# RWKV attention, soft MoE and FFN in one kernel: the low weights to GpSimd, the opening of the FFN in another order

## The chip, the cores and the metric

The kernel runs on one core of a Trainium2 chip. The metric is device microseconds of one launch; the median of three runs of the kernel before is 386.32 us (386.26 to 386.83).

## What is computed

Three layers follow each other. The first is a linear attention with a decaying state (4 batches, 8 heads, 768 tokens, head size 48), the second a soft mixture of 8 experts with 4 slots each, the third a feed-forward layer:

```python
y[t]   = r[t] @ (state + (u * k[t]) outer v[t]);  state = w * state + k[t] outer v[t]
logits = x @ phi;  d = softmax over tokens;  c = softmax over slots
slot_out[e] = relu((d.T @ x)[e] @ w1[e]) @ w2[e]
x2     = c @ slot_out                      # 3072 tokens x 384
h      = x2 @ w_in;  g = h * sigmoid(1.702 * h);  out = g @ w_out    # 384 -> 2048 -> 384
```

## The kernel before, in words

Each engine has its own instruction list, written out by hand; they meet only through semaphores, each of which counts up. An instruction that waits holds everything behind it on its engine. The first 120 us are the attention, in 6 chunks of 128 tokens by 4 batches; the experts follow until about 154 us; the rest is the FFN, which is what the change touches.

The FFN is not computed as `(c @ slot_out) @ w_in`. The 32 slot rows are first multiplied with `w_in`, which gives a matrix M of 2048 columns (spread over 128 rows as `mst`), and then `hidden(i, f)` (L569) is one 128x512 matmul of `mst`'s block f (128 of the 2048 hidden columns, 16 blocks) with the weights `ct` of token tile i (512 tokens, 6 tiles). The operands of the FFN's matmuls have the type fp32r; each is split into a high part (a copy in that type) and a low part (the difference to the fp32 value), and the products are summed. For each block f of each tile i:

- TensorE: `hidden(i, f)` writes bank f % 4.
- ScalarE: `sigmoid(i, f)` (L1046) writes `sg`.
- VectorE: `product(i, f)` (L850) multiplies bank and `sg` to `gf` (two buffers).
- ScalarE: `high(i, f)` (L1052) copies `gf` to `ghi`. VectorE: `low(i, f)` (L857) subtracts to `glo` (four buffers each).
- TensorE: `product(i, f)` (L576) adds nine matmuls to three output banks: `whi` x `glo`, `whi` x `ghi`, `wlo` x `ghi` for each of three column blocks m.

TensorE runs `LEAD` = 3 hidden blocks ahead of the product. ScalarE's list runs `sigmoid(f)` ahead of `high(f - 1)`, VectorE's `product(f)` ahead of `low(f - 1)`.

The output weight is split in the same way while tile 0 runs, in nine parts (`PARTS`, L36: blocks 0, 1, then pairs 2-3, 4-5 ... 14-15): `high_wout(part)` (L1034) on ScalarE writes `whi`, `low_wout(part)` (L872) on VectorE writes `wlo` from the loaded weight and `whi`. TensorE waits for `wlo_ok` ahead of the product of every even block of tile 0 (L649).

The opening of tile 0 is written out by hand (L604 to L644 on TensorE, L882 to L907 on VectorE, L1071 to L1095 on ScalarE). M of the first 256 columns is made first (L608) with its own high and low part (L1073, L885, `mf_ok`), so that `hidden(0, 0)` and `hidden(0, 1)` can go before the whole of M is there; then M of all columns (L613: three k, each of four column tiles; `m_ps` at the end), then a few warm-up matmuls (`keep_warm`, L331) and `opening()`, the product of block 0 with its `wlo` part last (L591). Four pairs of matmuls (L630, L631) spread M over the batches' rows; four copies turn them into `mst` in SBUF, quarters 0 and 2 on ScalarE (L1063, `mst_even`), quarters 1 and 3 on VectorE (L877, `mst_odd`). `hidden(0, 2)` follows, then `product(0, 1)` with `hidden(0, 3)` let in ahead of its last column block by the argument `within`, then `tile(0)` (L646) from f = 2: `hidden(0, f + 3)`, then `product(0, f)`.

GpSimd's last work before the change is `spr` (L1180), at 135.8 us.

Of the kernel before, what the change touches and what calls it, by code (L numbers as in the profile page):

```python
# [8 lines left out]
ALU = mybir.AluOpType  # L9
# [10 lines left out]
KD = DM // P  # L20
# [4 lines left out]
KF = FF // P  # L25
# [10 lines left out]
PARTS = ((0, 1), (1, 2)) + tuple((k, k + 2) for k in range(2, KF, 2))  # L36
# [5 lines left out]
LEAD = 3  # L42
# [3 lines left out]
def wait(eng, sem, value):  # L46

    if not isinstance(value, int) or value > 0:
        eng.wait_ge(sem, value)


def rwkv_soft_moe_ffn(nc, rk, kr, v, wcol, u, phi, w1, w2, win, wout, ident, strict, match, jsel, sel, parts, out):
    with ExitStack() as ctx:
        place = {"at": (nc.sbuf_base + 31) // 32 * 32}

        def sb(name, shape, dt=F32):
            size = 4
            for n in shape[1:]:
                size *= n
            t = nc.alloc_sbuf_tensor_at(name, shape, dt, offset=place["at"])  # L60
            place["at"] += (size + 31) // 32 * 32
            return t

        def sem(name):
            return ctx.enter_context(nc.semaphore(name))
# [91 lines left out]
        whi = sb("whi", [P, KF, DM], F32R)  # L157
        assert place["at"] == ring_at + 4 * SLOT_W * WLO_AT
        wlo = sb("wlo", [P, KF, DM], F32R)

        bank = [ctx.enter_context(nc.psum_tensor(f"bank{i}", [P, 512], F32)) for i in range(3)]
# [38 lines left out]
        own_ok, te_ps, spr_made, cturn_ps, chi_ok, clo_ok, mst_ps, mst_even, mst_odd = (  # L200
            sem(n) for n in ("own_ok", "te_ps", "spr_made", "cturn_ps", "chi_ok", "clo_ok", "mst_ps", "mst_even", "mst_odd"))
        rmax_ok, csub_ok, cexp_ok, rsum_ok, c_ok, ct_ps, ct_ok, whi_ok, wlo_ok = (
            sem(n) for n in ("rmax_ok", "csub_ok", "cexp_ok", "rsum_ok", "c_ok", "ct_ps", "ct_ok",
                             "whi_ok", "wlo_ok"))
# [12 lines left out]
        wraw = ring[:, WOUT_AT:WOUT_AT + 2, :].rearrange("p a n -> p (a n)").rearrange("p (k n) -> p k n", k=KF)  # L217
# [110 lines left out]
        def _(pe):  # L328
            pe.wait_ge(s_ident, 16)

            def keep_warm(to, count):  # L331

                for _ in range(count):
                    pe.matmul(to[:, 0:P], idt[:, :], idt[:, :], start=True, stop=True)  # L334
# [234 lines left out]
            def hidden(i, f):  # L569
                q = KF * i + f  # L570
                wait(pe, gf_ok, q - 3)
                pe.matmul(HB[f % 4][:, :], mst[:, f * P:(f + 1) * P],  # L572
                          ct_flat[:, bass.ds(i * TT, TT)],
                          start=True, stop=True).then_inc(hh_ps, 1)

            def product(i, f, within=None):  # L576
                q = KF * i + f
                pe.wait_ge(glo_ok, q + 1)
                hi, lo = ghi[:, f % 4, :], glo[:, f % 4, :]
                for m in range(KD):  # L580
                    if within and m == KD - 1:
                        within()
                    if f == 0:
                        wait(pe, o_ok, KD * (i - 1) + m + 1)
                    o = bank[4 + m][:, :]
                    w_hi, w_lo = whi[:, f, m * P:(m + 1) * P], wlo[:, f, m * P:(m + 1) * P]
                    pe.matmul(o, w_hi, lo, start=(f == 0), stop=False)  # L587
                    pe.matmul(o, w_hi, hi, start=False, stop=False)  # L588
                    pe.matmul(o, w_lo, hi, start=False, stop=(f == KF - 1)).then_inc(prod_ps, 1)  # L589
# [21 lines left out]
            for k in range(KD):  # L611
                for q in range(4):
                    last = pe.matmul(LG[32 * q:32 * q + 32, :], sot[:, k, :],  # L613
                                     win_sb[:, k, 512 * q:512 * q + 512], start=(k == 0), stop=(k == KD - 1))
                if k == 0:
                    pe.wait_ge(mf_ok, 1)
                    hidden(0, 0)
                    hidden(0, 1)
# [1 line left out]

            pe.wait_ge(ct_ok, B + 2)
            pe.wait_ge(spr_made, B)
            keep_warm(bank[2], 3)
            opening()
            pe.wait_ge(mhi_ok, 1)
            pe.wait_ge(mlo_ok, 1)
# [6 lines left out]
            pe.wait_ge(mst_odd, 1)  # L633
            hidden(0, 2)
            pe.wait_ge(wlo_ok, 2)

            def third():
                pe.wait_ge(mst_odd, 2)
                hidden(0, 3)

            product(0, 1, third)
            pe.wait_ge(mst_even, 2)
            for f in range(4, 2 + LEAD):
                hidden(0, f)  # L644

            def tile(i, more):  # L646
# [17 lines left out]
        def _(dve):  # L664
# [185 lines left out]
            def product(i, f):  # L850
                q = KF * i + f
                dve.wait_ge(sg_ok, q + 1)
                wait(dve, ghi_ok, q - 1)
                wait(dve, glo_ok, q - 1)
                dve.tensor_tensor(gf[:, f % 2, :], bank[f % 4][:, :], sg[:, f % 2, :], ALU.mult).then_inc(gf_ok, 1)  # L855

            def low(i, f):  # L857
                q = KF * i + f
                dve.wait_ge(ghi_ok, q + 1)
                wait(dve, prod_ps, KD * (q - 3))  # L860
                dve.tensor_tensor(glo[:, f % 4, :], gf[:, f % 2, :], ghi[:, f % 4, :], ALU.subtract)\  # L861
                   .then_inc(glo_ok, 1)
# [6 lines left out]
                    else:  # L869
                        low(i - 1, KF - 1)  # L870

            def low_wout(part):  # L872
                dve.wait_ge(whi_ok, part + 1)
                k = slice(*PARTS[part])
                dve.tensor_tensor(wlo[:, k, :], wraw[:, k, :], whi[:, k, :], ALU.subtract).then_inc(wlo_ok, 1)

            def copied(q):  # L877
                dve.wait_ge(mst_ps, q + 1)
                dve.tensor_copy(mst[:, 512 * q:512 * q + 512].rearrange("p (g k c) -> p g k c", g=2, k=2),
                                bank[MB[q]][:, :].rearrange("p (g c k) -> p g k c", g=2, k=2)).then_inc(mst_odd, 1)  # L880
# [3 lines left out]
            low_rows = mst[64:P, 0:FIRST].rearrange("p (k c) -> p k c", k=2)  # L884
            dve.scalar_tensor_tensor(low_rows, bank[5][64:P, 0:FIRST].rearrange("p (c k) -> p k c", k=2), rden[64:P, :],  # L885
                                     low_rows, ALU.mult, ALU.subtract).then_inc(mf_ok, 1)
            low_wout(0)
            low_wout(1)
            product(0, 0)
            product(0, 1)  # L890
            low(0, 0)
# [1 line left out]
            dve.scalar_tensor_tensor(mhl[:, 1, :], LG[:, :], rden, mhl[:, 0, :], ALU.mult, ALU.subtract)\  # L893
               .then_inc(mlo_ok, 1)
            low(0, 1)
            low_wout(2)
            copied(1)
            copied(3)
            product(0, 2)
            low(0, 2)  # L900
            low_wout(3)
            product(0, 3)
            for f in range(4, KF):
                product(0, f)
                low(0, f - 1)
                if f % 2 and f // 2 + 2 < len(PARTS):
                    low_wout(f // 2 + 2)  # L907
            with dve.Fori(1, C) as i:
                tile(i)
            low(C - 1, KF - 1)  # L910
# [3 lines left out]
        def _(act):  # L914
# [119 lines left out]
            def high_wout(part):  # L1034
                act.wait_ge(wout_in[PARTS[part][0] // QK], 16)
                k = slice(*PARTS[part])
                act.activation(whi[:, k, :], wraw[:, k, :], ACT.Copy).then_inc(whi_ok, 1)
# [8 lines left out]
            def sigmoid(i, f):  # L1046
                q = KF * i + f
                act.wait_ge(hh_ps, q + 1)
                wait(act, gf_ok, q - 1)
                act.activation(sg[:, f % 2, :], bank[f % 4][:, :], ACT.Sigmoid, scale=1.702).then_inc(sg_ok, 1)  # L1050

            def high(i, f):  # L1052
                q = KF * i + f
                act.wait_ge(gf_ok, q + 1)
                wait(act, prod_ps, KD * (q - 3))
                act.activation(ghi[:, f % 4, :], gf[:, f % 2, :], ACT.Copy).then_inc(ghi_ok, 1)  # L1056
# [6 lines left out]
            def copied(q):  # L1063

                g = slice(1 if q == 0 else 0, 2)
                act.wait_ge(mst_ps, q + 1)
                act.activation(mst[:, 512 * q:512 * q + 512].rearrange("p (g k c) -> p g k c", g=2, k=2)[:, g, :, :],
                               bank[MB[q]][:, :].rearrange("p (g c k) -> p g k c", g=2, k=2)[:, g, :, :], ACT.Copy)\
                   .then_inc(mst_even, 1)
# [11 lines left out]
            act.wait_ge(m_ps, 1)  # L1081
            act.activation(mhl[:, 0, :], LG[:, :], ACT.Copy, scale=rden).then_inc(mhi_ok, 1)
            high(0, 1)
            high_wout(2)
            copied(0)
            copied(2)
            sigmoid(0, 2)
            high(0, 2)
            high_wout(3)
            sigmoid(0, 3)  # L1090
            for f in range(4, KF):
                sigmoid(0, f)
                high(0, f - 1)
                if f % 2 == 0 and f // 2 + 2 < len(PARTS):
                    high_wout(f // 2 + 2)  # L1095
            with act.Fori(1, C) as i:
                for f in range(KF):
                    sigmoid(i, f)
# [83 lines left out]
                    .then_inc(spr_made, 1)  # L1182


# [57 lines left out]
```

## Time and profile before

| what | value |
|---|---|
| median of 3 runs | 386.32 us |
| profiled execution, its own time | 386.26 us |
| span of the profiled execution | 384.5 us |
| mean granted TensorE clock | 0.999 |
| TensorE busy | 373.3 us, 97% |
| VectorE busy | 234.3 us, 61% |
| ScalarE busy | 186.2 us, 48% |
| GpSimd busy | 96.4 us, 25%, none of it after 136 us |

The span is the part between the first and the last instruction of the one execution that the profiler took. The shares are averages over stages with different limits: attention, experts and FFN each have their own. A busy TensorE is not one at its peak, as the end of each matmul is modelled: two matmuls that lie 0.23 us apart are shown with 0.39 us each, and overlap.

### The profile page before, as it was taken

To read this page: it belongs to the slowest core of one execution; us is meant where nothing else is said; L and a number is where in the kernel's file an instruction comes from. 1 tells how busy PE (TensorE), PEld (TensorE's weight loads), DVE (VectorE), ACT (ScalarE), POOL (GpSimd) and SP (SyncE) were. 2 spreads that over 40 slices of the span, in tenths; PEclk is the share of its full clock that TensorE was granted. 3 is DMA by queue.
4 is the path that set the end of the run, shared out by engine and by line. 5 is a ranking of instruction groups with operands and counts; after the bars stand their busy time and mean duration, and the time that the engine had idled before them with its cause. 6 is when DMAs were issued, how large, how long until landed. Compare 5 with 4: busy or idle time off the path is not lost.

```text
span 384.5 us, 9081 instructions
## 1 busy us (share of the span) xinstructions
PE 373.3 (97%) x3220; PEld 292.9 (76%) x3220; DVE 234.3 (61%) x429; ACT 186.2 (48%) x410; POOL 96.4 (25%) x113
## 2 busy tenths in 40 slices
PE   7799999999999999999999999999999999999996
PEld 6678787887876344568888888888888888888885
DVE  6787878887784301678756555655565556655660
ACT  1235454545434441576564456445644464465552
POOL 5888788787672110000000000000000000000000
PEclk9999999999999999999999999999999999999999
DMA  7899999999999899700001002000200020002002
GB/s 231 292 328 396 397 389 398 388 363 368 401 356 414 349 377 413 274 0 3 0 27 57 0 2 82 0 0 0 82 0 0 0 82 0 0 0 82 0 2 82
DMA packets 21797, 63.76 MB, mean 166 GB/s; under 512 B 3088, under 2 KB 6816, under 8 KB 21392
## 3 DMA queue, kind: packets, MB, share of 16 engines
q1 hardware_dynamic: 20432, 62.99, 43.2%
q10 hardware_dynamic: 1344, 0.49, 0.7%
q8 instruction: 14, 0.23, 0.3%
q14 instruction: 7, 0.06, 0.0%
HBM read 58.75 MB, written 4.72 MB: 165 GB/s over the span
## 4 chain that ended last, share of the span: by engine, by line
PE 92%; POOL 3%; DVE 1%; issue 1%; ACT 1%; DMA 1%; DVEq 0%; POOLq 0%; ACTq 0%
PE bank L588 11%; PE bank L589 11%; PE bank L587 11%; PE bank L347 6%; PE pair L587 6%; PE pair L386 6%; PE pair L589 5%; PE pair L588 5%; PE bank L572 4%; PE pair L377 3%; PE pair L369 3%; PE bank L407 3%; PE bank L534 3%; PE bank L514 2%; PE bank L334 2%; PE bank L398 2%
## 5 line engine op out<-in xcount | busy, mean ns | idle before, releaser
L855 DVE TENSOR_TENSOR gf<-bank,sg 128x512 f32<-128x512 f32 x72 | 49.7, 691 | 59.1 <-ACT sg L1050 58.8
L1050 ACT ACTIVATE sg<-bank 128x512 f32<-128x512 f32 x72 | 42.9, 597 | 73.5 <-PE bank L572 73.5
L588 PE MATMUL bank<-ghi,whi 128*128 128x512 f32 x190 | 73.9, 389 | 0.0
L587 PE MATMUL bank<-glo,whi 128*128 128x512 f32 x190 | 73.9, 389 | 0.0
L589 PE MATMUL bank<-ghi,wlo 128*128 128x512 f32 x190 | 73.9, 389 | 0.0
L861 DVE TENSOR_TENSOR glo<-gf,ghi 128x512 fp32r<-128x512 f32 x96 | 66.3, 691 | 1.0 <-ACT ghi L1056 0.7
L1056 ACT ACTIVATE ghi<-gf 128x512 fp32r<-128x512 f32 x96 | 60.0, 625 | 2.0 <-DVE gf L855 1.9
L938 ACT ACTIVATE yt<-pair 112x512 f32<-112x512 f32 x24 | 14.3, 598 | 56.5 <-PE pair L386 56.5
L587 PEld LDWEIGHTS bank<-glo,whi 128*128 128x128 f32 x190 | 35.7, 188 | 7.4
L589 PEld LDWEIGHTS bank<-ghi,wlo 128*128 128x128 f32 x190 | 35.7, 188 | 7.4
L588 PEld LDWEIGHTS bank<-ghi,whi 128*128 128x128 f32 x190 | 35.7, 188 | 7.4
L587 PE MATMUL pair<-glo,whi 128*128 128x512 f32 x95 | 37.2, 391 | 0.5 <-DVE glo L861 0.4
L588 PE MATMUL pair<-ghi,whi 128*128 128x512 f32 x95 | 37.0, 389 | 0.0
L589 PE MATMUL pair<-ghi,wlo 128*128 128x512 f32 x95 | 37.0, 389 | 0.0
L727 DVE COPY_PREDICATED at<-keep,bank 128x512 f32<-128x512 int32 x48 | 32.4, 727 | 5.2 <-PE bank L347 4.8
L347 PE MATMUL bank<-rks 48*128 48x128 f32 x384 | 27.9, 284 | 3.5 <-DVE rks L708 2.5
L708 DVE TENSOR_TENSOR rks<-rkb,bank 112x512 f32<-112x512 f32 x48 | 30.4, 672 | 0.0
L855 DVE TENSOR_TENSOR gf<-pair,sg 128x512 f32<-128x512 f32 x24 | 16.6, 692 | 22.6 <-ACT sg L1050 22.4
L347 PEld LDWEIGHTS bank<-rks 48*128 48x128 f32 x384 | 23.4, 187 | 7.4 <-issue 3.4
L572 PE MATMUL bank<-ct,mst 128*128 (+1 forms) x72 | 27.9, 392 | 0.4 <-DVE mst L885 0.4
L1125 POOL TENSOR_TENSOR rkn<-krb 128x384 f32<-128x384 f32 x24 | 24.1, 1005 | 10.5 <-DMA krb<-kr 10.3
L386 PE MATMUL pair<-at,vb 128*48 128x128 f32 x384 | 25.9, 277 | 0.0
(176 smaller groups left out, 516.5 us busy)
## 6 DMA issues: line engine op xcount, KB each, us to landing
ring<-w SPq DMA_DIRECT2D x24, 512.0 KB, 6.2
rkb<-rk SPq DMA_DIRECT2D x23, 512.0 KB, 5.3
krb<-kr SPq DMA_DIRECT2D x24, 384.0 KB, 5.4
ring<-w SPq DMA_DIRECT2D x4, 1536.0 KB, 13.3
ring<-w SPq DMA_DIRECT2D x8, 768.0 KB, 8.9
vb<-v SPq DMA_DIRECT2D x24, 192.0 KB, 5.5
out<-ob SPq DMA_DIRECT2D x18, 256.0 KB, 2.1
ring<-win SPq DMA_DIRECT2D x3, 1024.0 KB, 14.7
```

The costliest lines, as they stand in the source:

```text
L347: last = pe.matmul(SC[i][:, hp * CH:(hp + 1) * CH], rks[s, b % 2, 1, hp, :], rks[s, b % 2, 0, hp, :], start=True, stop=True)
L386: last = pe.matmul(YT[i][o0:o0 + D, a * CH:(a + 1) * CH], vb[:, b, 2 * (a + 2 * w) + i, :], at[:, b % 2, i, a + 2 * w, :], start=False, st ...
L572: pe.matmul(HB[f % 4][:, :], mst[:, f * P:(f + 1) * P], ct_flat[:, bass.ds(i * TT, TT)], start=True, stop=True).then_inc(hh_ps, 1)
L587: pe.matmul(o, w_hi, lo, start=(f == 0), stop=False)
L588: pe.matmul(o, w_hi, hi, start=False, stop=False)
L589: pe.matmul(o, w_lo, hi, start=False, stop=(f == KF - 1)).then_inc(prod_ps, 1)
L708: dve.tensor_tensor(rks[a, b % 2, x, :, :], rkb[a, b % 2, x, :, :], w[a, :, :], ALU.mult)\
L727: dve.copy_predicated(at[:, b % 2, half, :, :], keep[:, :].unsqueeze(1).to_broadcast([P, 4, CH]), SC[half][:, :].rearrange("p (h t) -> p h ...
L855: dve.tensor_tensor(gf[:, f % 2, :], bank[f % 4][:, :], sg[:, f % 2, :], ALU.mult).then_inc(gf_ok, 1)
L861: dve.tensor_tensor(glo[:, f % 4, :], gf[:, f % 2, :], ghi[:, f % 4, :], ALU.subtract)\
L1050: act.activation(sg[:, f % 2, :], bank[f % 4][:, :], ACT.Sigmoid, scale=1.702).then_inc(sg_ok, 1)
L1056: act.activation(ghi[:, f % 4, :], gf[:, f % 2, :], ACT.Copy).then_inc(ghi_ok, 1)
```

## The change

Five edits. The low parts of the output weight (all nine) move from VectorE's list to the end of GpSimd's. On TensorE the first two blocks of hidden go after k = 1 of the M product, not after k = 0; seven warm-up matmuls stand where three stood; and `hidden(0, 3)` goes behind the whole of `product(0, 1)`, not inside it. On ScalarE the third part of `whi` goes between the two copies of M, `high(0, 2)` goes behind `high_wout(3)` and `sigmoid(0, 3)`, and the later parts go one block earlier. On VectorE `low(0, 2)` goes behind `product(0, 3)`.

```diff
@@ TensorE
-            def product(i, f, within=None):
+            def product(i, f):
...
-                    if within and m == KD - 1:
-                        within()
...
-                if k == 0:
+                if k == 1:
                     pe.wait_ge(mf_ok, 1)
                     hidden(0, 0)
                     hidden(0, 1)
...
-            keep_warm(bank[2], 3)
+            keep_warm(bank[2], 7)
             opening()
...
             hidden(0, 2)
             pe.wait_ge(wlo_ok, 2)
-
-            def third():
-                pe.wait_ge(mst_odd, 2)
-                hidden(0, 3)
-
-            product(0, 1, third)
+            product(0, 1)
             pe.wait_ge(mst_even, 2)
-            for f in range(4, 2 + LEAD):
+            pe.wait_ge(mst_odd, 2)
+            for f in range(3, 2 + LEAD):
                 hidden(0, f)
@@ VectorE
-            low_wout(0)
-            low_wout(1)
             product(0, 0)
             product(0, 1)
             low(0, 0)
...
             low(0, 1)
-            low_wout(2)
             copied(1)
             copied(3)
             product(0, 2)
-            low(0, 2)
-            low_wout(3)
-            product(0, 3)
-            for f in range(4, KF):
+            for f in range(3, KF):
                 product(0, f)
                 low(0, f - 1)
-                if f % 2 and f // 2 + 2 < len(PARTS):
-                    low_wout(f // 2 + 2)
@@ ScalarE
             high(0, 1)
+            copied(0)
             high_wout(2)
-            copied(0)
             copied(2)
             sigmoid(0, 2)
-            high(0, 2)
             high_wout(3)
-            sigmoid(0, 3)
-            for f in range(4, KF):
+            for f in range(3, KF):
                 sigmoid(0, f)
                 high(0, f - 1)
-                if f % 2 == 0 and f // 2 + 2 < len(PARTS):
-                    high_wout(f // 2 + 2)
+                if f % 2 and f // 2 + 3 < len(PARTS):
+                    high_wout(f // 2 + 3)
@@ GpSimd, at the end of its list
+            for part, blocks in enumerate(PARTS):
+                pool.wait_ge(whi_ok, part + 1)
+                k = slice(*blocks)
+                pool.tensor_tensor(wlo[:, k, :], wraw[:, k, :], whi[:, k, :], ALU.subtract).then_inc(wlo_ok, 1)
```

## Rows read from the trace of the kernel before

**Rows 1.** Windows, all engines: busy us (instructions), granted clock, DMA share, GB/s.
```profile
155.00:173.00 18.00, 17.12 (x101) 11.05 (x94) 12.88 (x20) 12.52 (x24) 0.00 (x0) 1.00 0.31 119
173.00:380.80 207.80, 207.80 (x919) 172.04 (x917) 121.96 (x186) 110.88 (x200) 0.00 (x0) 1.00 0.05 19
```
**Rows 2.** Timeline of TensorE: start us, us, line, out<-in, count, idle before and releaser.
```profile
155.84 1.04 PE L613 MATMUL bank<-ring,sot 128*32 128x512 f32 x8
157.27 0.50 PE L572 MATMUL bank<-ct,mst 128*128 128x512 f32 x1 [0.39 <-DVE mst L885]
157.94 1.92 PE L613 MATMUL bank<-ring,sot 128*32 128x512 f32 x16
159.79 0.94 PE L334 MATMUL bank<-idt 128*128 128x128 f32 x6
160.67 0.47 PE L596 MATMUL pair<-glo,whi 128*128 128x512 f32 x1
164.69 0.50 PE L572 MATMUL bank<-ct,mst 128*128 128x512 f32 x1
167.31 0.61 PE L572 MATMUL bank<-ct,mst 128*128 128x512 f32 x2
167.99 0.50 PE L587 MATMUL pair<-glo,whi 128*128 128x512 f32 x1
170.98 0.50 PE L587 MATMUL pair<-glo,whi 128*128 128x512 f32 x1 [0.43 <-DVE glo L861]
```
**Rows 3.** Timeline of ScalarE in the opening of the FFN.
```profile
156.53 0.93 ACT L1037 ACTIVATE whi<-ring 128x384 fp32r<-128x384 f32 x2
163.49 0.38 ACT L1067 ACTIVATE mst<-pair 128x256 fp32r<-128x256 f32 x1 [1.62 <-PE pair L631]
164.39 0.60 ACT L1067 ACTIVATE mst<-bank 128x512 fp32r<-128x512 f32 x1 [0.52 <-PE bank L631]
165.22 0.60 ACT L1050 ACTIVATE sg<-bank 128x512 f32<-128x512 f32 x1 [0.23 <-PE bank L572]
166.58 0.63 ACT L1056 ACTIVATE ghi<-gf 128x512 fp32r<-128x512 f32 x1 [0.76 <-DVE gf L855]
167.11 0.83 ACT L1037 ACTIVATE whi<-ring 128x768 fp32r<-128x768 f32 x1
167.85 0.58 ACT L1050 ACTIVATE sg<-pair 128x512 f32<-128x512 f32 x1
```
**Rows 4.** Timeline of VectorE in the opening of the FFN.
```profile
158.44 1.29 DVE L855 TENSOR_TENSOR gf<-bank,sg 128x512 f32<-128x512 f32 x2 [0.17 <-ACT sg L1050]
167.24 0.69 DVE L861 TENSOR_TENSOR glo<-gf,ghi 128x512 fp32r<-128x512 f32 x1 [0.70 <-ACT ghi L1056]
167.98 0.96 DVE L875 TENSOR_TENSOR wlo<-ring,whi 128x768 fp32r<-128x768 f32 x1
168.85 0.68 DVE L855 TENSOR_TENSOR gf<-pair,sg 128x512 f32<-128x512 f32 x1
```
**Rows 5.** Groups on GpSimd by shape: busy us, mean ns, idle before.
```profile
L1125 POOL TENSOR_TENSOR rkn<-krb 128x384 f32<-128x384 f32 x24 | 24.1, 1005 | 10.5 <-DMA krb<-kr 10.3
L1147 POOL TENSOR_TENSOR vd<-vb,dds 128x384 f32<-128x384 f32 x24 | 19.9, 829 | 4.0 <-DVE dds L715 4.0
L1172 POOL TENSOR_TENSOR lnat<-lnat,rm 128x640 f32<-128x640 f32 x1 | 1.3, 1265 | 1.8 <-DVE rm L754 1.8
```
**Rows 6.** Timeline: GpSimd and VectorE in the attention.
```profile
49.98 0.83 POOL L1147 TENSOR_TENSOR vd<-vb,dds 128x384 f32<-128x384 f32 x1
50.15 0.67 DVE L760 TENSOR_TENSOR stat<-stat 128x1 f32<-128x1 f32 x1
...
87.44 0.16 DVE L760 TENSOR_TENSOR stat<-stat 128x1 f32<-128x1 f32 x1
```
**Rows 7.** TensorE's longest wait after its start, and the window behind it.
```profile
17.76 1.16 PE L347 MATMUL bank<-rks 48*128 48x128 f32 x16 [1.74 <-DVE rks L708]
...
16.00:20.00 4.00, 2.26 (x32) 1.97 (x32) 3.20 (x7) 1.20 (x5) 3.92 (x5) 1.00 0.91 300
```

More of the change, by code:

```diff
@@ L870, in tile @@
                         low(i - 1, KF - 1)
[L872 to L875, printed above, removed]
             def copied(q):
```

## Prediction

> **What bounds the kernel now.** I read the windows first. From 173.0 to 380.8 us TensorE is busy for all of its time at a granted clock of 1.00 and issues 919 matmuls, one every 0.227 us; in the 18 us before that it is busy for 17.12 and the modelled ends hide more idle than that [rows 1]. After 173 us neither VectorE nor ScalarE nor GpSimd can therefore shorten anything, and 96 tiles of products run at TensorE's pace to the end. The change touches the opening of that stage, so the question is when the unbroken stream starts: I follow `hidden(0, 7)`, which goes out at about 173.2 us now, or `product(0, 4)` right behind it at 173.4 (both one product of 2.05 us behind the restart at 171.09). What that moment moves, the end moves.
>
> Second view, the timeline of TensorE alone [rows 2]. A row behind a wait begins with its weight load, 0.11 us ahead of the matmul (0.50 us instead of 0.39). The real stalls: `hidden(0, 0)` goes at 157.38, held by `mf_ok`; six warm-up records fill the time up to the opening at about 160.75; `product(0, 2)` goes at 168.10 behind the two hidden matmuls that end their issue at 167.77 (0.33 us lost, on `glo`); `product(0, 3)` goes at 171.09, where TensorE was free at 170.39 (0.70 us lost, on `glo`). Third, ScalarE and VectorE in the same stretch [rows 3, 4], to see which instruction in their queues makes `glo` late.
>
> Constants that I take from these rows: matmul issued to ScalarE or VectorE started, 0.43 us (164.79 to 165.22); `glo` end to the product's first matmul, 0.17 us (167.93 to 168.10); ScalarE's next start comes 0.48 us after a sigmoid's start, 0.53 after a `ghi`, 0.74 after a 768-wide `whi`; VectorE's comes 0.60 us after a 512-wide one, which lasts 0.69.
>
> **Part 1: one more block of the M product ahead of `hidden(0, 0)`.** Sixteen L613 records take 157.94 to about 159.7, in groups of four at 0.43 us, so one k costs 0.87 us [rows 2]. k = 0 starts at 155.84; with k = 1 behind it the two end at 157.57, and with the 0.09 us that the change of operand shape costs between 157.85 and 157.94 `hidden(0, 0)` goes at 157.66 instead of 157.38: +0.28 us (ends 0.19 and 0.4). The chain sigmoid, `gf`, `ghi`, `glo` behind it is all latency: `gf` of block 0 waited for ScalarE at 158.44, and VectorE had finished its two small `wlo` parts by then [rows 4]. Taking these parts off VectorE gives nothing here. The opening moves to 161.03. The seven warm-up matmuls are 14 records; the six now span 0.94 us with the last one's modelled length, some 0.115 us each, so 14 need 1.6 us from about 159.1 to 160.7: they fit in the wait, cost 0. Were that cover gone, each would cost 0.23.
>
> **Part 2: `wlo` on GpSimd.** GpSimd is empty in this stage [rows 1]. The trace has no 128x768 subtract there. Two plain 384-wide inputs take 1005 ns; with one broadcast input 384 takes 829 and 640 takes 1265, so 1.70 ns an element over a fixed 0.18 us; the plain form by the same fixed part is 2.15 ns an element and 1.83 us for 768. The upper end is two instructions of 1005, 2.01; the lower end is VectorE's own 0.96, with which part 4 would have ended before `low(0, 3)` and no hold is left [rows 4, 5]. I take 1.83, since it rests on the same operation on the same engine. Parts 0 and 1 (`whi` out at 157.04 and 157.46 [rows 3]) are there by 159.1 and wanted at 162.4 and 165.3. Part 2 is made later than now, as `high_wout(2)` stands behind `copied(0)`: that starts at 163.77, `whi` at 164.07, GpSimd from 164.97 to 166.8, wanted with `product(0, 2)` near 169.9. Nothing waits for GpSimd's output itself, with 3 us to spare at the closest.
>
> **Part 3: ScalarE's order.** `high_wout(2)` now pushes `copied(2)` to 164.81, which ends at 165.4; it is wanted at 167.4, and `sigmoid(0, 2)` waits for its matmul until 165.50 in any case (165.22 plus 0.28). Cost 0. The costly edit is the next one: `high(0, 2)` stood directly behind `sigmoid(0, 2)`; now `high_wout(3)` and `sigmoid(0, 3)` are ahead of it, and on VectorE `product(0, 3)` is ahead of `low(0, 2)`. `sigmoid(0, 3)` needs `hidden(0, 3)`, and on TensorE that no longer stands inside `product(0, 1)` but behind all nine of its matmuls. So: `product(0, 1)` at 165.30, `hidden(0, 3)` at 165.30 + 2.05 = 167.35, `sigmoid(0, 3)` 167.78, `high(0, 2)` 168.26, `gf` of block 3 168.41, `low(0, 2)` 169.01 to 169.70, `product(0, 2)` at 169.87. TensorE has only the hidden matmuls 3, 4 and 5 to put into this and is through at 168.03: a stall of 1.84 us where 0.33 stood. The shift grows from 0.28 to 1.77 us. Then something comes back: `product(0, 2)` and `hidden(0, 6)` last until 172.15, and `glo` of block 3 (ScalarE: `whi` 168.79, sigmoid 4 169.53, `ghi` 170.01; VectorE: `gf` of 4 170.16, `low(0, 3)` 170.76 to 171.45) would be in time. The old stall of 0.70 is gone; shift 172.15 - 171.09 = +1.06.
>
> **Part 4: VectorE beside GpSimd.** This is where the relief of VectorE turns round. `low` reads two SBUF tensors. The trace has such VectorE instructions beside GpSimd only in a tiny form: `negn` (L760, one element) takes 0.16 us alone and 0.67 when GpSimd is inside `vd`, and ends at 50.82 where GpSimd's ends at 50.81 [rows 6]. So a VectorE instruction with two SBUF inputs waited for the end of GpSimd's. `gf` has only one SBUF input and is not in question. If the same holds for 512 elements, `low` ends at best 0.55 us behind GpSimd's instruction (0.02, and 0.53 that its length of 0.69 has over 0.16). GpSimd's part 4 follows its `whi` from 169.69 to 171.52 and meets `low(0, 3)`: that ends at 172.07, `product(0, 3)` goes at 172.24, +0.09. Part 5 follows its `whi` (ScalarE 171.55 to 172.39) from 172.45 to 174.28 and meets `low(0, 4)`, due at 172.58: that ends at 174.83, `product(0, 4)` goes at 175.00 where TensorE was free at 174.52, +0.48. Behind that `low` runs over 2 us ahead of its product, and a hold of up to 1.3 us costs nothing. With 2.01 us for GpSimd the two come to 0.75 instead of 0.57, without any hold to 0.
>
> The Trainium skill speaks against this change in the same sense: "SBUF — State Buffer", section "SBUF: two separate sides", calls the port pair of VectorE and GpSimd an exclusive lock that the first to start keeps for a whole instruction, for a VectorE operation with two SBUF inputs against a GpSimd one that reads SBUF. The one-element rows agree in when they end; that a `low` which starts first keeps GpSimd waiting is not in this trace. By the rule the sum is 1.63, by the length that `low` has now (0.69 throughout) 1.06. The Trainium skill's "GPSIMD Engine Reference", section "Elementwise — side-by-side cycle accounting", gives 4497 ns for a 2048-wide `tensor_tensor` add on GpSimd; scaled to 768 that is an estimate of 1.7 us, by which the sum would be 1.5; no row here has that operation.
>
> **Sum.** 0.28 + 1.49 - 0.71 + 0.09 + 0.48 = +1.63 us. The profiled execution took 386.26 us for a span of 384.5; with 1.63 more it is 387.9. The median of the runs shown is 386.32, so the forecast is 387.9 by either.
>
> **Rivals.**
> A, the forecast: order stall and hold, 387.9 (387.5 to 388.3). 0.52.
> B, the order stall alone: 387.3. For it: only one-element operands show the hold, and the meeting with part 5 hangs on 0.13 us (172.45 against 172.58); if `low(0, 4)` is first, the sum is 1.15. 0.25.
> C, holds go on: GpSimd and VectorE keep meeting, and each of parts 4 to 8 costs what part 5 does, 1.06 + 5 x 0.48 = 3.5, 389.8; smaller versions lie between. Against it: from block 5 on `glo` has 2 us of lead. 0.08.
> D, faster: the VectorE queue decides. Now `low_wout(3)` sits between `low(0, 2)` and `gf` of block 3, whose sigmoid ended at 168.43 while it began at 168.85 [rows 3, 4]; without it the chain is 0.39 us earlier, the stall of 0.70 shrinks, and the time is 385.9. It decides if `ghi` of block 2 does not really come behind `sigmoid(0, 3)`, that is if `hidden(0, 3)` were out by 165.6, so that its sigmoid falls into the gap on ScalarE. The program order speaks against it. 0.06.
> E, in between: no hold and the first shift of 0.28 not felt, 0.78, 387.0. 0.09.
>
> **Numbers.** What a measurement here can tell from no change is 0.2%, 0.77 us, so up to 387.1. A, B and C are slower: 0.85. E is the same: 0.09. D is faster: 0.06. The range takes A and B whole and the near part of C: 387.1 to 388.8.
>
> **What would show it.** In the profile after: `hidden(0, 0)` 0.2 to 0.4 us later; a TensorE wait of some 1.8 us ahead of `product(0, 2)` put down to `glo`, with `high(0, 2)` behind `sigmoid(0, 3)`; 128x768 subtracts on GpSimd of 1.8 to 2.0 us; single `low` rows of 1.3 to 2.3 us that end with GpSimd's, the rest at 0.69; a second wait ahead of `product(0, 4)`; then no idle to the end. I am wrong if the wait ahead of `product(0, 2)` is under 1 us, if TensorE shows idle behind 177 us, or if its granted clock drops in the stall (which I price at nothing: 1.74 us of idle before 17.76 us left it at 1.00 [rows 7]).

## The result and the profile after

| | kernel before | changed kernel |
|---|---|---|
| median of 7 runs, side by side | 387.05 us | 388.98 us (387.99 to 389.63) |
| ratio, 95% interval | | 1.0051 (1.0032 to 1.0072), slower by 0.5% |
| profiled execution: time, span | 386.26, 384.5 us | 389.18, 387.4 us |
| mean granted TensorE clock in it | 0.999 | 0.991 |
| first M matmul (L608, now L606) | 154.52 us | 155.62 us |
| last product matmul | 380.78 us | 383.69 us |
| between the two | 226.26 us | 228.07 us |

The change is slower, as forecast, but the time of 388.98 lies 0.18 us above the range, and the move is 2.0 us (1.2 to 2.8) where 1.6 was forecast. The profile splits the 2.9 us of the two executions in two parts: 1.10 us are lost before the first line that the change touches, 1.81 us behind it. I use the last line of the table throughout, since it leaves out the first part. Two kernels that differ in the start alone agree in it within 0.05 us (226.26 and 226.21, 228.07 and 228.07 below), so it shows tenths in a single execution. Its two ends in the kernel before are these; those of the changed kernel are the first and the last row of the timeline below.

```profile
154.52 1.50 PE L608 MATMUL bank<-ring,sot 128*32 128x256 f32 x24
...
380.78 0.39 PE L589 MATMUL bank<-ghi,wlo 128*128 128x512 f32 x1
```

The timeline of TensorE in the changed kernel, which answers to [rows 2]:

```profile
155.62 1.50 PE L606 MATMUL bank<-ring,sot 128*32 128x256 f32 x24
156.94 1.90 PE L611 MATMUL bank<-ring,sot 128*32 128x512 f32 x16
158.77 0.73 PE L572 MATMUL bank<-ct,mst 128*128 128x512 f32 x2
...
160.43 1.83 PE L334 MATMUL bank<-idt 128*128 128x128 f32 x14
...
166.17 0.50 PE L572 MATMUL bank<-ct,mst 128*128 128x512 f32 x1
...
168.82 0.61 PE L572 MATMUL bank<-ct,mst 128*128 128x512 f32 x2
170.99 0.50 PE L585 MATMUL pair<-glo,whi 128*128 128x512 f32 x1 [1.56 <-DVE glo L855]
...
173.43 0.47 PE L585 MATMUL pair<-glo,whi 128*128 128x512 f32 x1
...
176.14 0.50 PE L585 MATMUL pair<-glo,whi 128*128 128x512 f32 x1 [0.19 <-DVE glo L855]
...
383.69 0.39 PE L587 MATMUL bank<-ghi,wlo 128*128 128x512 f32 x1
```

Take 1.10 off each start to compare it with before. `product(0, 2)` begins at 169.89 instead of 167.99, behind a wait that the row gives as 1.56 us. Without the modelled end of the last hidden matmul it is more: that was issued at 169.05, TensorE was free at 169.28, and the product's first matmul went at 171.10 (0.11 behind its weight load), 1.82 us. `product(0, 3)` has a wait of about 0.1, `product(0, 4)` of 0.46.

ScalarE, then VectorE, in the same stretch (they answer to [rows 3, 4]): `high(0, 2)` at 169.51 now stands behind `sigmoid(0, 3)` at 169.02, which had waited 0.98 us for its matmul; and two of VectorE's `low` rows are long.

```profile
164.97 0.38 ACT L1048 ACTIVATE mst<-pair 128x256 fp32r<-128x256 f32 x1 [2.59 <-PE pair L629]
165.25 0.84 ACT L1018 ACTIVATE whi<-ring 128x768 fp32r<-128x768 f32 x1
165.99 0.59 ACT L1048 ACTIVATE mst<-bank 128x512 fp32r<-128x512 f32 x1
166.70 0.60 ACT L1031 ACTIVATE sg<-bank 128x512 f32<-128x512 f32 x1
167.20 0.84 ACT L1018 ACTIVATE whi<-ring 128x768 fp32r<-128x768 f32 x1
169.02 0.60 ACT L1031 ACTIVATE sg<-pair 128x512 f32<-128x512 f32 x1 [0.98 <-PE pair L572]
169.51 0.62 ACT L1037 ACTIVATE ghi<-gf 128x512 fp32r<-128x512 f32 x1
```

```profile
169.65 0.69 DVE L849 TENSOR_TENSOR gf<-pair,sg 128x512 f32<-128x512 f32 x1 [1.62 <-ACT sg L1031]
170.25 0.68 DVE L855 TENSOR_TENSOR glo<-gf,ghi 128x512 fp32r<-128x512 f32 x1
...
171.99 1.35 DVE L855 TENSOR_TENSOR glo<-gf,ghi 128x512 fp32r<-128x512 f32 x1
173.48 0.69 DVE L849 TENSOR_TENSOR gf<-bank,sg 128x512 f32<-128x512 f32 x1
174.09 2.00 DVE L855 TENSOR_TENSOR glo<-gf,ghi 128x512 fp32r<-128x512 f32 x1
```

GpSimd's subtracts, which the trace of before could only show for other shapes and meetings [rows 5, 6]:

```profile
170.94 1.86 POOL L1167 TENSOR_TENSOR wlo<-ring,whi 128x768 fp32r<-128x768 f32 x1 [1.00 <-ACT whi L1018]
173.69 1.85 POOL L1167 TENSOR_TENSOR wlo<-ring,whi 128x768 fp32r<-128x768 f32 x1 [0.89 <-ACT whi L1018]
178.38 2.25 POOL L1167 TENSOR_TENSOR wlo<-ring,whi 128x768 fp32r<-128x768 f32 x1 [2.85 <-ACT whi L1018]
```

`low(0, 3)` ends at 173.34, GpSimd's part 4 at 172.80; `low(0, 4)` ends at 176.09, part 5 at 175.54: 0.54 and 0.55 us behind, the 0.55 of the forecast.

The part that the change does not touch, in windows of the changed kernel's execution at the start (the columns are those of [rows 1], the clock is the third from the right):

```profile
10.00:12.00 2.00, 0.92 (x9) 0.73 (x7) 2.00 (x4) 0.49 (x1) 1.57 (x2) 1.00 1.10 344
12.00:14.00 2.00, 1.15 (x10) 1.15 (x12) 0.80 (x2) 0.00 (x0) 1.92 (x3) 0.71 0.60 218
14.00:16.00 2.00, 2.00 (x16) 1.43 (x14) 1.47 (x3) 0.00 (x0) 2.00 (x4) 0.50 0.94 321
16.00:18.00 2.00, 2.00 (x26) 1.97 (x28) 1.59 (x3) 0.11 (x1) 1.92 (x2) 0.50 0.97 332
18.00:20.00 2.00, 2.00 (x29) 1.88 (x24) 0.91 (x2) 1.38 (x5) 1.46 (x3) 0.58 0.74 185
```

and the scores' matmuls in TensorE's timeline there:

```profile
12.85 2.08 PE L347 MATMUL bank<-rks 48*128 48x128 f32 x16 [1.94 <-DVE at L721]
...
18.41 1.75 PE L347 MATMUL bank<-rks 48*128 48x128 f32 x16
...
23.01 1.16 PE L347 MATMUL bank<-rks 48*128 48x128 f32 x16 [0.36 <-DVE rks L702]
```

TensorE had idled for 1.94 us; the granted clock fell to 0.5 (1.2 instead of 2.4 GHz) near 12.8 us and rose again near 19.7, as the shares of 0.71 and 0.58 in their windows give it. Sixteen matmuls took 2.08 us instead of 1.16. The third batch of scores starts at 18.41 where it started at 17.76 before [rows 7], the fourth at 23.01 where it was 21.81: 1.2 us, and the FFN begins 1.10 us late.

### The profile page after: what moved, and what is told of

It reads as the page before. It is cut to its first block, busy times and chain, and to the rows that moved or that the text cites. A ratio compares the mean times of both kernels' runs of the same rounds, so it can differ in the third digit from the quotient of the medians.

```text
span 387.4 us, 9097 instructions
## 1 busy us (share of the span) xinstructions
PE 376.3 (97%) x3228; PEld 295.5 (76%) x3228; DVE 230.4 (59%) x420; ACT 186.2 (48%) x410; POOL 111.8 (29%) x122
## 4 chain that ended last, share of the span: by engine, by line
PE 92%; DVE 3%; DMA 2%; issue 1%; ACT 1%; SPq 0%; POOL 0%; DVEq 0%; POOLq 0%; ACTq 0%
PE bank L587 11%; PE bank L586 11%; PE bank L585 11%; PE bank L347 7%; PE pair L386 6%; PE pair L585 6%; PE pair L587 5%; PE pair L586 5%; PE bank L572 4%; PE pair L369 4%; PE pair L377 3%; PE bank L407 3%; PE bank L534 3%; PE bank L514 2%; PE bank L398 2%; DMA vb<-v 2%
## 5 line engine op out<-in xcount | busy, mean ns | idle before, releaser
L855 DVE TENSOR_TENSOR glo<-gf,ghi 128x512 fp32r<-128x512 f32 x96 | 69.1, 720 | 0.2
L347 PE MATMUL bank<-rks 48*128 48x128 f32 x384 | 29.4, 295 | 2.6 <-DVE at L721 1.9
L347 PEld LDWEIGHTS bank<-rks 48*128 48x128 f32 x384 | 24.7, 197 | 6.4 <-DVE at L721 2.1
L386 PE MATMUL pair<-at,vb 128*48 128x128 f32 x384 | 26.8, 283 | 0.0
```

The source lines that it names most:

```text
L347: last = pe.matmul(SC[i][:, hp * CH:(hp + 1) * CH], rks[s, b % 2, 1, hp, :], rks[s, b % 2, 0, hp, :], start=True, stop=True)
L386: last = pe.matmul(YT[i][o0:o0 + D, a * CH:(a + 1) * CH], vb[:, b, 2 * (a + 2 * w) + i, :], at[:, b % 2, i, a + 2 * w, :], start=False, st ...
```

## The experiments

**warm_before and warm_after: is the loss at the start the change's?**

```diff
-                    keep_warm(LG, 4)
+                    keep_warm(LG, 9)
...
                         state(*prev(c, b))
+                    if is_first(c, b - 1):
+                        keep_warm(LG, 6)
```

> Kernel before with 9 instead of 4 warm-up matmuls behind the transposes of the first scores and 6 more behind the first state, so that TensorE's two waits near 11 and 16 us are filled. Theory 1 (the 1.1 us that the changed kernel's profile had lost before the FFN come from a granted clock of 0.5 between 13 and 19 us, which an execution gets or not, whatever the kernel): granted clock 1.00 between 8 and 20 us, times close together at 386.2 to 386.6. Rival (the loss came with the change itself, or with the load of the chip): times scatter as those of the kernel before, 386.3 to 387.5, and a mean clock of 0.991 or 0.995 still turns up.

> Changed kernel with the same filled waits. The span from the first M matmul (L606) to the last product matmul was 226.26 us before and 228.07 after, so theory 1 expects this kernel 1.8 us above warm_before (388.0 to 388.4), with little scatter and clock 1.00; the rival expects 388.0 to 389.6 as without the filling, and 2.5 us or more above.

The mean clock of all 12 runs of each was 0.999 or 1.00. The kernel before had run 35 times beside them: 386.07 to 388.45 us, median 387.55, with a mean clock under 0.998 in 24 of 35. Its 11 runs with the full clock have a median of 386.63 (386.07 to 388.36), the other 24 of 387.8 (386.45 to 388.45): with the fall the median is 1.1 us higher, though the two groups overlap. In a later set on another chip it came in 6 of 17 runs. The changed kernel was the same: in 11 of its 19 runs the clock was low (388.12 to 389.97), in 8 full (387.57 to 390.78, median 388.10). So an execution has the fall or has not, in either kernel, and TensorE's idle near 11 and 16 us lets it in: with the idle filled it did not come in 24 runs, nor in 12 of late_parts below.

The profiles of all the runs say the same. Four have a fall, and in them TensorE had idled for 1.94, 1.83, 1.77 and 2.07 us just before it (the changed kernel, k_back, memset_only, parts_back); in the six without a fall whose idle was not filled, the longest one there was 1.44 to 1.74 us. What a fall costs depends on where it lies: the fourth batch of scores starts at 23.01, 21.75, 22.09 and 23.09 us in those four, and at 21.39 to 21.83 us in the nine without one.

Medians: warm_before 386.87 (386.46 to 387.59), warm_after 388.78 (387.75 to 389.67), 1.91 us apart; from the first M matmul to the last product matmul 226.21 and 228.07. So the difference between the two kernels is there without any fall, and the loss at the start is not the change's. The forecast times were missed all the same: both medians lie above what the theory gave (386.2 to 386.6, and 388.0 to 388.4), and the scatter that is left, 1.1 us in warm_before and 1.9 us in warm_after, is about what the rival gave. What decides against the rival is the clock, and the 1.91 us where it gave 2.5 or more.

The rest of the scatter is not the clock's, as it shows in profiles at full clock: the FFN starts between 154.3 and 155.4 us in them. The traces place most of it between the eighth and the ninth batch of scores, near 45 us. That distance is 4.16 to 5.30 us; from the ninth batch to the first M matmul all 13 profiles take 110.0 to 110.1 us. GpSimd stands there for 1.5 to 3.4 us in every profile, and the trace puts that down to a load (`krb`). In the ten profiles without the filler the FFN starts 111.5 to 111.8 us behind the end of that wait, which comes at 42.8 us in the earliest and at 44.7 in the latest. Why the load lands at different times stays open.

The windows of warm_before over the same stretch:

```profile
8.00:12.00 4.00, 4.00 (x44) 3.76 (x43) 1.96 (x4) 0.82 (x2) 3.26 (x4) 1.00 1.07 373
12.00:16.00 4.00, 3.81 (x61) 3.33 (x59) 2.47 (x5) 0.11 (x1) 3.92 (x5) 1.00 0.76 228
16.00:20.00 4.00, 4.00 (x54) 3.53 (x50) 3.19 (x7) 1.39 (x5) 3.92 (x5) 1.00 0.91 301
```

The Trainium skill, "TensorE: Matmul & The Clock Gate", section "Part 1: The HAM clock gate (the "warmup" mystery)", says that the moment at which a TensorE that starts slow gets its full clock varies from run to run. What varies from run to run here is the fall: over 35 executions of one kernel the mean clock lies between 0.989 and 1.00.

**gp_only: the low parts on GpSimd, nothing else.** Kernel before without its five places of `low_wout`, and with the changed kernel's loop at the end of GpSimd's list.

> Kernel before with one edit: all nine low parts on GpSimd, nothing else moved. Span from the first M matmul to the last product matmul, 226.26 before: theory (VectorE's low waits for the end of a GpSimd subtract): 226.26 + 0.32 = 226.6, with two or three low rows of 1.3 to 2.0 us and waits ahead of product(0,4) and product(0,5). Rival (VectorE is only relieved): 226.26 - 0.37 = 225.9, all low rows 0.69.

226.56 us. VectorE and GpSimd show where the 0.37 of relief went:

```profile
168.32 0.69 DVE L855 TENSOR_TENSOR gf<-pair,sg 128x512 f32<-128x512 f32 x1 [0.52 <-ACT sg L1044]
...
171.54 1.36 DVE L861 TENSOR_TENSOR glo<-gf,ghi 128x512 fp32r<-128x512 f32 x1
173.03 0.69 DVE L855 TENSOR_TENSOR gf<-bank,sg 128x512 f32<-128x512 f32 x1
173.64 1.99 DVE L861 TENSOR_TENSOR glo<-gf,ghi 128x512 fp32r<-128x512 f32 x1
```

```profile
170.49 1.85 POOL L1182 TENSOR_TENSOR wlo<-ring,whi 128x768 fp32r<-128x768 f32 x1 [0.74 <-ACT whi L1031]
173.23 1.84 POOL L1182 TENSOR_TENSOR wlo<-ring,whi 128x768 fp32r<-128x768 f32 x1 [0.89 <-ACT whi L1031]
```

`gf` of block 3 is earlier than in [rows 4], as rival D had it, and then `low(0, 4)` and `low(0, 5)` are held behind GpSimd's parts. TensorE's two waits come to 0.31 us ahead of `product(0, 3)`, 0.70 in the kernel before, and there are new ones of 0.21 and 0.44 ahead of `product(0, 4)` and `product(0, 5)`. Ten runs, median 387.08, ratio 1.0002 (0.9982 to 1.0023): no difference that this measurement can tell.

**after_timed and gp_timed: the same subtracts, started elsewhere.** One line more in GpSimd's loop of the changed kernel, and another in that of gp_only.

```diff
                 pool.wait_ge(whi_ok, part + 1)
+                wait(pool, glo_ok, (0, 0, 0, 0, 4, 5, 8, 10, 12)[part])    # after_timed
+                wait(pool, glo_ok, (0, 0, 0, 3, 5, 7, 9, 11, 13)[part])    # gp_timed
```

> Changed kernel with one edit: GpSimd's parts 4 to 8 also wait for glo of blocks 3, 4, 7, 9 and 11, so that each starts behind the low that it had held. Theory: the holds ahead of product(0,3) and product(0,4) go, 228.07 - 0.60 = 227.5 from first M matmul to last product matmul; the stall of 1.9 us ahead of product(0,2) stays. Rival (the waits ahead of product(0,3) and (0,4) come from the order, not from GpSimd): 228.1 as before.

> gp_only with GpSimd's parts 3 to 8 also waiting for glo of blocks 2, 4, 6, 8, 10 and 12, so that a held low has a spare block's time ahead of its product. First M matmul to last product matmul, 226.26 before and 226.56 in gp_only: theory (moving the low parts alone gains 0.37 us by relieving VectorE ahead of gf of block 3, and the holds took 0.69 of it back): 225.9. Rival (the relief is worth nothing): 226.26 or more.

227.50 and 225.83 us, both as the theory had it. Ten timed runs of after_timed have a median of 388.47, ratio 1.0023 (1.0006 to 1.0040) to the kernel before. The holds have not gone, they have moved. In after_timed `low(0, 3)` is free, and `low(0, 4)` is held by a part that starts 0.6 us ahead of it:

```profile
171.79 0.68 DVE L855 TENSOR_TENSOR glo<-gf,ghi 128x512 fp32r<-128x512 f32 x1
...
173.22 1.81 DVE L855 TENSOR_TENSOR glo<-gf,ghi 128x512 fp32r<-128x512 f32 x1
```

but with no wait ahead of `product(0, 3)` it still ends 0.5 us before its product goes. In gp_timed `low(0, 5)` is held (173.14 to 174.95) and its product goes at 175.31, without a wait. A hold costs only where the product behind it is due before the hold ends.

**memset_only: does any GpSimd instruction hold `low`?**

```diff
+            pool.wait_ge(so_ps, 2)
...
-                pool.tensor_tensor(wlo[:, k, :], wraw[:, k, :], whi[:, k, :], ALU.subtract).then_inc(wlo_ok, 1)
+                if part < 4:
+                    pool.tensor_tensor(wlo[:, k, :], wraw[:, k, :], whi[:, k, :], ALU.subtract).then_inc(wlo_ok, 1)
+                else:
+                    wait(pool, tables, part - 4)
+                    pool.memset(rks[:, :, :, :, :], 0.0).then_inc(tables, 1)
+                    pool.memset(wlo[:, k, :].bitcast(F32), 0.0).then_inc(wlo_ok, 1)
```

> Changed kernel in which GpSimd's parts 4 to 8 only write: each subtract is replaced by a memset of 2048 unused elements and one of the part (so the low part of the weight of blocks 6 to 15 is left out, zero). GpSimd is busy longer than before (1.8 + 0.7 us a part) but reads nothing. Theory 1 (VectorE's low waits for GpSimd instructions that read SBUF): no low row above 0.7 us, 228.07 - 0.60 = 227.5. Theory 2 (it waits for any GpSimd instruction that is under way): low rows of 1.3 to 2 us as in the changed kernel, about 228.1.

227.42 us, and the longest of all 96 `low` rows is 0.694 us, although GpSimd was busy with memsets throughout `low(0, 3)` and `low(0, 5)`, the two shown:

```profile
170.03 1.82 POOL L1172 MEMSET rks<- 128x2048 f32 x1 [0.95 <-ACT whi L1018]
171.77 0.75 POOL L1173 MEMSET wlo<- 128x768 f32 x1
172.77 1.81 POOL L1172 MEMSET rks<- 128x2048 f32 x1 [0.25 <-ACT whi L1018]
```

```profile
171.10 0.68 DVE L855 TENSOR_TENSOR glo<-gf,ghi 128x512 fp32r<-128x512 f32 x1
...
173.94 0.68 DVE L855 TENSOR_TENSOR glo<-gf,ghi 128x512 fp32r<-128x512 f32 x1
```

So GpSimd being under way is not enough; the subtract, which reads two tensors, holds, and the memsets, which only write, do not. No run has a GpSimd instruction other than the subtract that reads beside a `low`. The clause "only against a GpSimd op that reads SBUF" in the Trainium skill ("SBUF — State Buffer", section "SBUF: two separate sides") agrees with these rows.

**order_back and k_back: the order of ScalarE and VectorE, and the earlier M block, each undone in the changed kernel.**

```diff
@@ order_back, ScalarE and VectorE
             sigmoid(0, 2)
+            high(0, 2)
             high_wout(3)
+            sigmoid(0, 3)
...
-                if f % 2 and f // 2 + 3 < len(PARTS):
-                    high_wout(f // 2 + 3)
+                if f % 2 == 0 and f // 2 + 2 < len(PARTS):
+                    high_wout(f // 2 + 2)
...
             product(0, 2)
+            low(0, 2)
+            product(0, 3)
@@ k_back, TensorE
-                if k == 1:
+                if k == 0:
...
-            keep_warm(bank[2], 7)
+            keep_warm(bank[2], 3)
```

> Changed kernel with high(0,2) and low(0,2) back in front of sigmoid(0,3) and product(0,3), the whi parts at their old blocks; TensorE's order, the earlier M block and GpSimd's low parts stay as changed. First M matmul to last product matmul, 228.07 in the changed kernel: theory (the stall ahead of product(0,2) is made by ghi of block 2 standing behind a sigmoid whose matmul comes after all of product(0,1)): 227.0, with the wait ahead of product(0,2) back at 0.3 to 0.4 us although hidden(0,3) still goes late. Rival (TensorE's own order makes it): 228.1, wait of 1.9 us.

> Changed kernel with hidden(0,0) and (0,1) back behind k = 0 of the M product and three warm-up matmuls. Theory (the second M block shifts the whole opening by what it lasts): 228.07 - 0.39 = 227.7, hidden(0,0) 2.75 us behind the first M matmul instead of 3.15. Rival (the shift is absorbed later): 228.1.

226.94 and 227.67 us. In order_back `hidden(0, 3)` still goes behind all of `product(0, 1)`, at 167.28, `high(0, 2)` at 166.75 ahead of it, and `product(0, 2)` begins at 168.16 behind a wait of 0.3 us, as in the kernel before:

```profile
167.50 0.61 PE L572 MATMUL bank<-ct,mst 128*128 128x512 f32 x2
168.16 0.50 PE L585 MATMUL pair<-glo,whi 128*128 128x512 f32 x1
```

So the later place of `hidden(0, 3)` costs nothing by itself. In the changed kernel `high(0, 2)` stands behind `sigmoid(0, 3)`, which waits 0.98 us for that matmul. order_back undoes three edits at once (`high(0, 2)`, `low(0, 2)`, the later `whi` parts); no run tells them apart, and none keeps the changed order with `hidden(0, 3)` back inside `product(0, 1)`.

In k_back `hidden(0, 0)` goes 2.75 us behind the first M matmul, in the changed kernel it was 3.15.

**parts_back: the changed order without GpSimd.** The changed kernel with `low_wout` in VectorE's list again.

> Changed kernel with the low parts back on VectorE, the rest as changed. There low_wout(2) waits in front of copied(1) for a whi part that ScalarE now makes only behind copied(0). Theory: that delays copied(1) and hidden(0,2) by 1.6 us, and the stall ahead of product(0,2) of 1.9 us stays, while no low is held: 226.26 + 2.7 = 229.0, more than the 228.07 of the changed kernel. Rival (GpSimd is the whole of the loss): 227.5 or less.

228.97 us. `copied(1)` waits behind `low_wout(2)`, and TensorE for `copied(1)`, ahead of the stall that was there:

```profile
168.28 0.50 PE L572 MATMUL bank<-ct,mst 128*128 128x512 f32 x1 [1.44 <-DVE mst L873]
...
173.09 0.50 PE L585 MATMUL pair<-glo,whi 128*128 128x512 f32 x1 [1.56 <-DVE glo L855]
```

So in this order GpSimd saves 0.9 us on balance, holds and all, because it takes `low_wout(2)` out of VectorE's way to `copied(1)`; in the order of before it cost 0.3 (gp_only). The order makes the larger part of the loss: 1.51 of the 1.81 us lie between gp_only and the changed kernel.

**late_parts and late_no6: a version that beats both.** `whi` and `wlo` of part p are wanted with block 2(p - 1), and were made two to three blocks ahead of it, where part 3 stood between ScalarE's and VectorE's work for blocks 2 and 3.

```diff
@@ ScalarE and VectorE (both kernels)
-            high_wout(3)
...
-                if f % 2 == 0 and f // 2 + 2 < len(PARTS):
-                    high_wout(f // 2 + 2)
+                if f % 2 == 0 and f // 2 + 1 < len(PARTS):
+                    high_wout(f // 2 + 1)
...
-            low_wout(3)
...
-                if f % 2 and f // 2 + 2 < len(PARTS):
-                    low_wout(f // 2 + 2)
+                if f % 2 == 0 and f // 2 + 1 < len(PARTS):
+                    low_wout(f // 2 + 1)
@@ TensorE (late_parts alone, with the filled waits of warm_before)
                     if f + LEAD < KF:
-                        hidden(i, f + LEAD)
+                        if not first or f != 3:
+                            hidden(i, f + LEAD)
+                        if first and f == 2:
+                            hidden(0, 6)
```

> A version that may beat both: kernel before with the filled waits of warm_before, parts 3 to 8 of whi and wlo made one to one and a half blocks later (behind high(0,3), (0,5) ... on ScalarE and low(0,3), (0,5) ... on VectorE, none on GpSimd), and hidden(0,6) in front of product(0,2). Theory (the 1.03 us of stalls ahead of product(0,2) and product(0,3) come from whi and wlo part 3 in the queues in front of sigmoid and gf of block 3): 226.2 - 0.95 = 225.3 from first M matmul to last product matmul, 1 us less than warm_before. Rival (the stalls are latency of the chain hidden, sigmoid, gf, ghi, glo): 226.0 or more.

> late_parts without the early hidden(0,6) and without the filled waits at the start: kernel before with parts 3 to 8 of whi and wlo one to one and a half blocks later, nothing else. Theory: the stall of 0.70 us ahead of product(0,3) goes and the 0.33 ahead of product(0,2) stays, 226.26 - 0.72 = 225.5; so of the 0.9 us of late_parts 0.7 are the parts and 0.2 hidden(0,6). Rival (hidden(0,6) does the work): 226.0.

225.36 and 225.58 us. TensorE has no wait left ahead of `product(0, 3)`; in late_parts:

```profile
168.16 0.84 PE L574 MATMUL bank<-ct,mst 128*128 128x512 f32 x3
168.84 0.48 PE L589 MATMUL pair<-glo,whi 128*128 128x512 f32 x1
...
170.76 0.40 PE L591 MATMUL bank<-ghi,wlo 128*128 128x512 f32 x1
170.99 0.40 PE L589 MATMUL pair<-glo,whi 128*128 128x512 f32 x1
```

Timed over 12 runs, late_parts has a median of 386.04 us (384.86 to 387.33) against 386.67 of the kernel before beside it: ratio 0.9975 (0.9957 to 0.9992), a gain of 0.25% and the lowest median of the timed kernels. It has the filled waits too, so this ratio is not that of the parts alone; for them late_no6 gives 0.68 us between the two marks, in one execution, and `hidden(0, 6)` 0.22 more.

## Why the prediction was wrong, and where it was right

The forecast was slower by 1.6 us to 387.9. The direction and the mechanism in the FFN held, with each of its steps and one term too small; the time fell out of the range by the base on which the sum was put.

- **The base.** "The median of the runs shown is 386.32, so the forecast is 387.9 by either" is the step that failed. Of the three runs behind that median (386.26 to 386.83) the profiled one had the full clock (0.999); the clocks of the other two are not on record. Beside the changed kernel the kernel before has a median of 387.05, over 35 runs one of 387.55, and 24 of these have the fall. 1.8 us on top of 387.05 is 388.9. Of the seven timed runs of the changed kernel five have the fall, and the two without it took 387.99 and 388.65, inside the range, as is the median of all its eight runs at full clock, 388.10. The fall is the part of the base that is shown. The other part is the 1 us of scatter at full clock: warm_after has a median of 388.78 without any fall, at the edge of the range. In the profiles that scatter goes with a load that lands early or late, and why it does stays open. The range was built from the bounds of the FFN's terms alone, with none for the start. The prediction looked at that place, "1.74 us of idle before 17.76 us left it at 1.00 [rows 7]", and read one execution as a rule: the same kind of idle, 1.77 to 2.07 us, was followed by the fall in four others. The stall that the change itself makes did leave the clock at 1.00.
- **Part 1**, "+0.28 us (ends 0.19 and 0.4)": 0.40 by k_back and by the rows (158.77 where 157.27 was, less 1.10), the upper end. From the first of the sixteen M records to the matmul of `hidden(0, 0)` it took 1.94 us (156.94 to 158.88); the forecast had 1.82 (155.84 to 157.66), with 0.09 for the change of shape and nothing for the 0.11 us by which the weight load stands ahead of the matmul. This is the one term that was mis-sized, by 0.12 of the 0.18 us that lie between 1.63 and the measured 1.81; the other 0.06 I can give to no term. The seven warm-up matmuls fitted: the opening moved by 0.39, as `hidden(0, 0)` did.
- **Part 2**: GpSimd's subtract takes 1.83 to 1.87 us where I took 1.83 (one of 2.25 is told below), the small ones 1.00, and nobody waited for its output.
- **Part 3**: the wait ahead of `product(0, 2)` is 1.82 us, forecast 1.84; undoing its cause gave back 1.13 (order_back). The forecast's own terms for it are 1.49 - 0.71 = 0.78; the rest is the relief of VectorE ahead of `gf` of block 3 (0.43 by gp_timed), which the changed order leaves no room for, less 0.1 that the holds then cost more (0.64 us in order_back, 0.54 in the changed kernel).
- **Part 4**: holds of `low(0, 3)` and `low(0, 4)` with the lengths and ends forecast; on TensorE 0.1 and 0.46 us, forecast 0.09 and 0.48. Taking their cost away in three ways (after_timed, memset_only, gp_timed against gp_only) gave 0.57, 0.65 and 0.73. The lead of over 2 us that the prediction gave `low` behind these was less at first: `glo` was ready 1.05, 1.9 and 1.9 us ahead of its product for blocks 5 to 7.
- **The rivals.** B (no hold) is out by the long rows, and E (no hold, first shift not felt) by them and by k_back. C is out by its price: the holds do go on (`low(0, 7)` takes 1.19 us), but from `product(0, 5)` on TensorE has no wait. D's mechanism exists and is worth 0.43 us, but only if the order stays and GpSimd's parts are started so that no product is due behind a held `low` (gp_timed, 225.83 against 226.26).
- **A count.** The "96 tiles of products" that run behind 173 us are 92: 6 tiles of 16 blocks, less the first four. The 919 matmuls of the row, ten for each, say the same, and nothing in the sum rests on it.

## What to carry to other kernels

Before adding a forecast to a base, ask how the base scatters: this kernel, whose TensorE idles for 1 to 2 us at a time soon after its start, runs with or without a fall of the clock, and a median of three runs lay 1.2 us below that of 35. Work moved to an idle engine is not off the path if it shares something with the engine that it relieves; see when it starts against the instructions it can hold, and whether the work behind these is due. And in lists written by hand, a step that is needed later (here `whi` and `wlo`) belongs behind the one that is needed now: moving it one block back gained 0.68 us (late_no6), moving its low half to another engine, at the better of the two sets of times tried in that order, 0.43 (gp_timed).

## What the hardware showed beside that

- The hold works both ways. Part 6 on GpSimd began at 178.38 while `low(0, 6)` ran (178.25 to 178.93) and lasted 2.25 us, 0.40 more than the others; it then held `low(0, 7)` from 180.00 to 181.19. The Trainium skill ("SBUF — State Buffer", section "SBUF: two separate sides") says that whoever starts first keeps the port pair for the whole instruction. The rows agree in both directions, though for GpSimd the 0.40 us is less than the 0.55 for which the two overlapped.
- `gf`, with one input in PSUM and one in SBUF, was never held: 0.69 us in every row beside a subtract on GpSimd.
- An idle of 1.94 us at 11 us was followed by the half clock for some 7 us; one of 1.82 us at 169 us in the same execution was not.
